# Attention head loop: the transposes of a tile split around score, value and turning products on TensorE

## The reference

```python
q_assign = argmax(einsum('bhsd,hcd->bhsc', q_n, c_n)); k_assign = ...   # 16 clusters
mask = q_assign[:, :, :, None] == k_assign[:, :, None, :]
scores = where(mask, q @ k.T / sqrt(64), -1e9)      # 16 heads (2 x 8), 768 x 768, head size 64
attn = softmax(scores);  x = attn @ v               # then x as (1536, 512) rows
x = moe(x, w_gate, w1, w2)                          # top-1 of 8 experts, relu
out = ((x @ w_a) * (x @ w_b)) @ w_out
```

## Time and profile before

| | |
|---|---|
| median of 3 runs | 807.0 us (806.86 to 807.27) |
| the profiled execution's own time | 807.03 us |
| its span | 805.3 us |
| PE busy | 795.0 us, 99% of the span |
| DVE, ACT, POOL busy | 459.5, 360.3, 365.3 us |
| granted TensorE clock | 0.999 of full speed (2.4 GHz) |

### The profile page before, as it was taken

The page is one execution under the profiler, slowest core; times in us unless marked ns, Lnnn a source line. Parts: engine busy times, 40 slices in busy tenths (PEclk is TensorE's granted clock), DMA queues, the critical chain, the costliest instruction groups (busy, mean ns, idle before and its releaser), DMA issues.

```text
span 805.3 us, 13176 instructions
## 1 busy us (share of the span) xinstructions
PE 795.0 (99%) x4412; PEld 674.8 (84%) x4413; DVE 459.5 (57%) x716; ACT 360.3 (45%) x740; POOL 365.3 (45%) x311
## 2 busy tenths in 40 slices
PE   8999999999999999999999999999999999999997
PEld 5899999999997688888888888888888888888886
DVE  5888988988997989999867004531212122121211
ACT  7877877877886444344443443211212111121112
POOL 6798898898891355454454634000411002010001
PEclk9999999999999999999999999999999999999999
DMA  7473463463342577888677314300101000010001
GB/s 205 111 193 95 110 181 94 112 178 95 76 127 74 171 237 220 246 250 258 217 216 227 105 39 107 117 0 14 32 8 53 1 14 13 1 53 0 1 1 52
DMA packets 48665, 86.62 MB, mean 108 GB/s; under 512 B 17856, under 2 KB 19904, under 8 KB 48624
## 3 DMA queue, kind: packets, MB, share of 16 engines
q1 hardware_dynamic: 41888, 69.36, 29.9%
q0 software_dynamic: 3856, 11.33, 4.9%
q10 hardware_dynamic: 2880, 5.39, 1.8%
HBM read 73.29 MB, written 11.30 MB: 105 GB/s over the span
## 4 chain that ended last, share of the span: by engine, by line
PE 77%; issue 17%; DVE 2%; DMA 2%; POOL 1%; ACT 1%; SPq 0%; POOLq 0%; DVEq 0%
PE bank L1733 9%; PE bank L1663 9%; PE bank L1464 7%; PE bank L1632 7%; PE bank L1630 7%; PE bank L1631 7%; PE bank L1670 4%; PE bank L1737 4%; PE bank L1480 4%; PE bank L1431 4%; PE bank L1452 4%; PE bank L1482 3%; PE bank L1504 2%; PE bank L1677 2%; PE bank L1391 2%
## 5 line engine op out<-in xcount | busy, mean ns | idle before, releaser
L1355 DVE TENSOR_TENSOR ab_raw<-bank,a_sb 128x512 f32<-128x512 f32 x35 | 24.2, 691 | 183.9 <-PE bank L1632 178.1
L409 DVE CAST w_split<-stage 128x1024 fp32r<-128x1024 f32 x68 | 70.0, 1029 | 68.2 <-PE bank L1670 52.7
L846 ACT ACTIVATE pT_hi<-bank 128x384 fp32r<-128x384 f32 x192 | 85.6, 490 | 43.7 <-PE bank L1464 42.9
L1096 DVE TENSOR_TENSOR pT_lo<-bank,pT_hi 128x384 fp32r<-128x384 f32 x192 | 98.9, 550 | 8.9 <-ACT pT_hi L846 8.5
L1128 DVE TENSOR_REDUCE neg_max<-bank 128x1 f32<-128x768 f32 x96 | 91.5, 954 | 19.6 <-PE bank L1452 19.0
L413 DVE TENSOR_TENSOR w_split<-stage,w_split 128x1024 fp32r<-128x1024 f32 x72 | 99.3, 1382 | 2.3
L717 POOL TENSOR_TENSOR hT_lo<-hT_raw,hT_hi 128x512 fp32r<-128x512 f32 x38 | 54.6, 1439 | 77.9 <-ACT hT_raw L921 77.8
L1464 PE MATMUL bank<-ident,probs 128*128 128x128 f32 x576 | 89.4, 276 | 0.3
L866 ACT ACTIVATE probs<-bank,neg_max 128x768 f32<-128x768 f32 x96 | 87.0, 906 | 3.4 <-DVE neg_max L1128 3.3
L981 ACT ACTIVATE a_sb<-bank 128x512 f32<-128x512 f32 x35 | 20.9, 597 | 131.9 <-PE bank L1632 123.2
L1733 PE MATMUL bank<-w_split,hT_hi 128*128 (+1 forms) x304 | 79.5, 403 | 0.0
(11 more groups left out here) (269 smaller groups left out, 1761.9 us busy)
## 6 DMA issues: line engine op xcount, KB each, us to landing
stage<-w SPq DMA_DIRECT2D x64, 512.0 KB
q_raw<-qT SPq DMA_DIRECT2D x32, 192.0 KB, 3.7
k_raw<-kT SPq DMA_DIRECT2D x32, 192.0 KB, 3.9
sorted_y<-y_sb ACTq DMA_DIRECT2D x19, 257.0 KB, 4.9
q_pair<-qT SPq DMA_DIRECT2D x8, 384.0 KB, 4.3
v_raw<-v_keys SPq DMA_DIRECT2D x16, 192.0 KB, 3.7
stage<-w_a SPq DMA_DIRECT2D x6, 512.0 KB
stage<-w_b SPq DMA_DIRECT2D x6, 512.0 KB
```

The costliest lines, as they stand in the source:

```text
L846: act.activation(pT_hi[:, half, part * GT:(part + 1) * GT, j * P:(j + 1) * P], pT_ps[part].rearrange("p (k q) -> p k q", q=P), ACT.Copy).t ...
L1096: dve.tensor_tensor(pT_lo[dst], pT_ps[part].rearrange("p (k q) -> p k q", q=P), pT_hi[dst].bitcast(F32), ALU.subtract).then_inc(s_pl, 1)
```

## The change

The numbers of lines in the changed kernel are two to nine larger from L1091 on. The change does four things:

1. The turnings are no longer issued after the six transposes of tiles 1 and 4 but one ahead of each of the three transposes of part 1.
2. In the same tiles the high score products of the next tile stand between part 0 and part 1 of the transposes; tiles 2 and 5 then have only their low ones.
3. In tiles 2 and 5 the first four of the six value products stand between the transposes' parts, and the two of key tile 2 behind part 1. They wait for one part less of `s_pl`.
4. VectorE does `scale_x` between part 0 and part 1 of `pT_lo` in tiles 1 and 4 instead of at the tile's end, behind a step of the cluster choice.

In the first pair the similarity products move from part 1 to part 0 in tiles 2 to 4.

```diff
-            def evacuate(n, qt, pT_ps=pT_ps):
+            def evacuate(n, qt, pT_ps=pT_ps, parts=range(2)):
                 half, j = qt // GT, qt % GT
-                for part in range(2):
+                for part in parts:
...
-                    if before or qt >= 2:
+                    if before and qt % GT == 1:
+                        evacuate(n - 2, (qt - 2) % QT, parts=(0,))
+                        scale_x(g - 1, pp - 1 + slot, 1 - slot, qt // GT)
+                        evacuate(n - 2, (qt - 2) % QT, parts=(1,))
+                    elif before or qt >= 2:
                         evacuate(n - 2, (qt - 2) % QT)
...
-                    if before and qt % GT == 1:
-                        scale_x(g - 1, pp - 1 + slot, 1 - slot, qt // GT)
...
-            def transpose_probs(n, slot, pT_ps=pT_ps, pp=None, first_sim=(None, None)):
+            def transpose_probs(n, slot, pT_ps=pT_ps, pp=None, first_sim=(None, None), back=None, next_high=None, values=None):
                 pe.wait_ge(s_exp, n + 1)
                 for part, done in ((0, s_TA), (1, s_TB)):
+                    if values is not None and part == 1:
+                        probs_v(*values, (0, 1))
+                    if next_high is not None and part == 1:
+                        pe.wait_ge(s_exp, n + 2)
+                        score_high(*next_high)
...
                     for j in range(QT // 2):
                         kt = part * (QT // 2) + j
+                        if back is not None and part == 1:
+                            turn_back_tile(*back, j)
...
             def probs_v(g, slot, half, key_tiles, oT_ps=oT_ps, pp=None, first_sim=None):
                 if key_tiles[0] == 0:
-                    pe.wait_ge(s_pl, 2 * (g * QT + (half + 1) * GT))
+                    pe.wait_ge(s_pl, 2 * (g * QT + (half + 1) * GT) - 1)
...
+            def turn_back_tile(g, half, j, x_ps=x_ps, o_T=o_T):
+                if j == 0:
+                    pe.wait_ge(s_oT, 2 * g + half + 1)
+                    if static(g) and g == 0 and half == 0:
+                        pe.wait_ge(s_bw, 4)
+                w = back_w[:, bass.ds(g, 1), :].rearrange("p g w -> p (g w)")
+                done = pe.matmul(x_ps[:, j, :], o_T[:, j * P:(j + 1) * P], w, start=True, stop=True)
+                if j == GT - 1:
+                    done.then_inc(s_back, 1)
...
-                sims_by_transposes = ({2: (None, 3), 3: (None, 6), 4: (None, 9)} if first else
+                sims_by_transposes = ({2: (3, None), 3: (6, None), 4: (9, None)} if first else
                                       {0: (None, 0), 1: (6, None), 2: (None, 9)}) if sim else {}
                 for qt in range(QT):
                     n = g * QT + qt
-                    score(pp, g, n, slot, qt)
+                    turning = before and qt % GT == 1
+                    score(pp, g, n, slot, qt, high=not (before and qt % GT == 2))
                     if before or qt >= 2:
-                        transpose_probs(n - 2, qt % 2, pp=pp + 1, first_sim=sims_by_transposes.get(qt, (None, None)))
+                        values = (g, slot, 0) if qt == QT - 1 else (g - 1, 1 - slot, 1) if before and qt == 2 else None
+                        transpose_probs(n - 2, qt % 2, pp=pp + 1, first_sim=sims_by_transposes.get(qt, (None, None)),
+                                        back=(g - 1, qt // GT) if turning else None,
+                                        next_high=(g, slot, qt + 1) if turning else None, values=values)
...
-                    if before and qt % GT == 1:
-                        turn_back(g - 1, qt // GT)
                     if before and qt == 2:
-                        probs_v(g - 1, 1 - slot, 1, range(GT))
+                        probs_v(g - 1, 1 - slot, 1, (2,))
...
                     if qt == QT - 1:
-                        probs_v(g, slot, 0, range(GT))
+                        probs_v(g, slot, 0, (2,))
```

More of the change, by code:

```diff
@@ L1431, in score_high, with score @@
                     pe.matmul(scores[qt % 2][:, lo:hi], q_hh[:, slot, at], k_hl[:, slot, lo:hi], start=True, stop=False)
-            def score(pp, g, n, slot, qt):
-                if not static(n) or n >= 2:
+            def score(pp, g, n, slot, qt, high=True):
+                if high and (not static(n) or n >= 2):
                     pe.wait_ge(s_exp, n - 1)
@@ L1496, in last_probs_v @@
                           start=False, stop=True).then_inc(s_pv, 1)
+            def turn_back_tile(g, half, j, x_ps=x_ps, o_T=o_T):
[7 more added lines that the diff above has]
+                    done.then_inc(s_back, 1)
             def turn_back(g, half, x_ps=x_ps, o_T=o_T):
-                pe.wait_ge(s_oT, 2 * g + half + 1)
-                if static(g) and g == 0 and half == 0:
-                    pe.wait_ge(s_bw, 4)
-                w = back_w[:, bass.ds(g, 1), :].rearrange("p g w -> p (g w)")
                 for j in range(GT):
-                    last = pe.matmul(x_ps[:, j, :], o_T[:, j * P:(j + 1) * P], w, start=True, stop=True)
-                last.then_inc(s_back, 1)
+                    turn_back_tile(g, half, j, x_ps, o_T)
             def head(pp, slot):
```

## The result

| | before | after |
|---|---|---|
| median | 807.05 us (806.86 to 807.27) | 814.95 us (814.68 to 815.21) |
| ratio | | 1.0097 (95% interval 1.0085 to 1.0109) |
| profiled execution, its span | 807.03, 805.3 us | 815.0, 813.2 us |

The change makes the kernel 7.9 us slower. The forecast was 811.4 with a range to 814.5: the direction is right, the size is not, and the measured time lies just above the range.

The account below looks back on a forecast made before the run. TensorE, busy 795.0 of 805.3 us, was taken to bound the kernel. Loop pairs 1.34 lost against 0.81 gained, six times +0.5, first pair +0.3, last +1.1: +4.4 us, 811.4 us, range 808.0 to 814.5.

Parts of the forecast that it names:

- Gain 1: Turnings between transposes on TensorE, tiles 1 and 4: 0.177 instead of 0.224 each, 4.2 us over 30 tiles.
- rival B: Alternation gains nothing: turnings still cost 0.224, waits give back a third of the missing 4.2 us; 814 us, chance 0.08.
- Gain 2: Value products of tile 5, even heads of the loop: scale_x comes earlier and their wait of 0.3 us goes.
- Place one: Transposes of tile 0 in odd heads wait for VectorE's late pT_lo: 0.35 and again 0.14, together 0.49 us.
- Place two: High products in tile 4 of odd heads wait for ScalarE's exponent of tile 3, late behind hot_rows: 0.46 us.
- the small waits: TensorE waits in a pair's other tiles, including 0.14 in even tile 0 and 0.06 in tile 2; 0.39 us in sum.
- Even heads 0.25 shorter: Sign to look for: even heads of the loop come out 0.25 us shorter than before.
- Odd heads, 0.8 longer: Sign to look for: odd heads of the loop 0.8 us longer; the forecast is wrong if they are not longer.
- First pair +0.3: First pair of heads: only two tiles with turnings, low parts late in head 1 by the choice's steps; +0.3 us.
- last pair +1.1: Last pair, no similarity products to give time: waits in heads 14, 15 and behind the last tile, against 4 x 0.14; +1.1 us.
- Rival A: The second part's lateness ends in VectorE's idle time in the loop, so only gains are left: 801 us, chance 0.13.
- C: It balances: half of the two large waits, 1.34 becomes 0.87 a pair; within 0.2% of before, chance 0.10.

Follow-up runs that it names:

- e6: Kernel after with change 1 undone: the three turnings again behind the six transposes; 815.38 us.
- e5: Kernel before with change 4 alone: VectorE does scale_x between the two parts of pT_lo in tiles 1 and 4; 810.36 us, ratio 1.0039.
- e3: Kernel after with ScalarE making the mask rows in tile 3 of odd heads instead of tile 2; 813.35 us.
- e1: Kernel after with the first similarity product's two register waits ahead of the wait for pT_lo in tile 0 of even heads; 814.45 us.
- e2: Kernel after with the whole first similarity product ahead of the wait for pT_lo in tile 0 of even heads; 812.56 us.
- e10: Kernel after with VectorE's scale_x waiting for the turned rows last, its other three counts first; 814.19 us.
- e11: Kernel after with both edits: first similarity product ahead of the wait for pT_lo, and scale_x waiting for the turned rows last; 812.03 us.
- e4: Kernel before with the cluster choice's steps in even heads of the loop in tiles 2, 2, 3, 5 instead of 2, 3, 4, 5; 805.43 us.
- e9: Kernel after with the cluster choice's steps in even heads of the loop in tiles 2, 2, 3, 5 instead of 2, 3, 4, 5; 815.66 us.

## Why the prediction was wrong, point by point

- **What bounds the kernel, and the stretch behind attention:** right.
- **Gain 1:** right as a price (0.29 for a pair; tile 1 of the even head 0.14 shorter once the 0.08 of the reading is put back), so rival B falls, though its 814 us lies nearest to the result: its time is near by luck, its condition is not met. The Trainium skill, "TensorE: Matmul & The Clock Gate", section "LDWEIGHTS (loading the stationary operand)", gives one load time for any 128 columns. The trace disagrees, with 0.29 for a turning and a transpose where 0.224 and 0.11 would make 0.33. What rival B got wrong besides is how much the waits give back, a third of the 4.2 us: e6 shows nearly all of it.
- **Gain 2:** right (tile 5 of even heads 0.18 shorter, 0.26 with the correction), but e5 shows that the edit which gets it costs 3.1 us by itself.
- **Place one, 0.49:** right; 0.52 (2.92 against 2.40), of it 0.32 ahead of the first transpose (121.68 to 122.35, less 0.35), where I had 0.35. **Place two, 0.46:** right in what is waited for; the wait is 0.34 (0.67 less three transposes' 0.33), tile 4 0.27 longer, 0.35 corrected, where 0.46 less 0.14 was forecast. e3 confirms the mask rows.
- **The step that failed is the small waits, "0.14 at the second transposes of tile 0 of the even head, 0.06 in its tile 2", part of the 0.39.** Measured: 0.37 in tile 0 and 0.20 in tile 2 (3.22 less 2.94, less 0.08), 0.37 more a pair, 2.2 us in six pairs. I let each wait end with 0.05 of semaphore and 0.06 of load, as if only the waiting product stood behind it. In tile 0 the count came 0.04 after the load was due, and the load 0.37 after. e1, e2 and e10 show what was missing: the queue instructions that carry waits and compute addresses, three at TensorE and two at VectorE, 0.1 us each. "Even heads 0.25 shorter" became 0.08 longer. With both put out of the way (e11) the kernel takes 812.03, 0.6 above 811.4, and 2.9 of the 3.5 us that were missed are gone; some of that is the small waits themselves, which were forecast.
- **Odd heads, 0.8 longer:** 0.93 to 0.98. The 0.15 lies mostly in tiles 1 and 5 and was not taken apart; its cause is open.
- **First pair +0.3, last pair +1.1:** the traces give +0.45 and about +1.05. The profiled execution's first low products came at 15.43 us, against 15.03 before; in the traces of the twelve experiments they come anywhere from 15.04 to 15.67, 15.59 in e4 with the old order on TensorE and 15.10 in e9 with the new one, so these 0.4 us do not follow the change.
- **Rival A** (the queues take it up) falls by places one and two, **C** by the same, as neither wait is halved. The bounds of 20 ns an operation and half or twice the semaphore gave +2.5 to +7; the result, +7.9, needed an instruction that was in no term.

With the loop at 6 x 1.0, the first pair 0.45, the last 1.05 and the start's 0.4, the sum is 7.9 us, the difference of the two profiled executions' spans.

## What to carry to other kernels

When an in-order engine is made to wait in a new place, count everything that its queue holds between that wait and the next useful instruction, register computations for waits and addresses included: 0.1 us each here, free until the wait is late. A count that was 0.04 us late cost 0.37. So put the wait that is released last nearest to the work that needs it, and put work that does not need it ahead of it.

Where three engines hand each other a tile, a saving on one of them that is paid with lateness of another need not be a gain: undone alone, it came back here to within 0.4 of 4.2 us. Try the smallest dose first (one turning instead of three), and look whether the wait that is to be cured can be taken away in the queue of the engine that is late; here it was a table of steps, worth 1.8 us. The same table cost 0.7 us in the kernel after (e9), so an edit's worth holds for the order of queues in which it was measured.

## What the runs showed of the hardware

- Queue instructions of TensorE and VectorE that compute a register or wait for a semaphore follow each other at 0.08 to 0.1 us when nothing covers them (106.175, 106.270, 106.367, load at 106.467; VectorE 111.838, 111.940, product at 112.024).
- Whether a wait is an instruction of its own changed with its neighbours: in the kernel after the wait for `pT_lo` was carried by a register instruction, in e1 by a semaphore instruction. Moving two waits saved one instruction, not two.
- A float32 product of two passes and a transpose behind it cost 0.29 us in alternation, with 72 columns as with 32. Transposes in a row start 0.11 apart, and three turnings in a row cost 0.224 each.
